# Attention without hi/lo splits: fp32 score matmuls of 64 rows, fp32 value product, three score tiles

## The chip, the cores and the metric

The kernel runs on one core of one Trainium2 chip. The metric is the time of one execution on the device in microseconds (us), lower is better. A core has five engines that run side by side and meet only at semaphores: TensorE (PE in the profile, its weight loads PEld), VectorE (DVE), ScalarE (ACT), GpSimd (POOL) and SyncE (SP), which here only issues the transfers. Matmuls write to PSUM, which has 8 banks; everything else lives in SBUF.

## The reference

```python
# q, k, v: (4 batches, 8 heads, 576 tokens, 64), fp32; tau = 0.02
scores = scale * q @ k.T                              # per batch and head, 576 x 576
thresh = max(scores, axis=-1) - tau
scores = where(scores >= thresh, scores, -1e9)
attn   = exp(scores - max(scores)); attn = attn / (sum(attn) + 1e-9)
x      = attn @ v                                     # -> 2304 tokens x 512
x      = (h - tanh(h)) @ w_out,   h = x @ w_in        # 512 -> 2048 -> 512
out    = (h * sigmoid(h)) @ w_out2, h = x @ w_in2     # 512 -> 2048 -> 512
```

The threshold compares scores with their row's maximum less 0.02, so the scores have to be good to nearly full fp32.

## The kernel before

There are two stages: attention, and then the two feed-forward layers. The feed-forward code (`hidden`, `project`, `chunk`) is the same in both kernels.

**Attention.** The 32 heads are taken in 16 pairs. The two heads of a pair have 2 x 576 query rows, which make nine tiles of 128 rows: eight whole ones (j = 0 to 7, alternately of head 0 and head 1) and a shared one (j = 8) with the last 64 rows of both. Four pairs make a batch of 36 tiles. The code is a software pipeline: each engine has a function `steps`, in which step k does tile k - lag of each kind of work, with lags that are constants (`L_S` = 8 for scores, maximum, statistics and exp; `L_MASK` = 9 for the threshold; `L_NORM` = 11; `L_T` = 13 for transposes; `L_LO` = 14; `L_PV` from 21 for the value product). Each engine runs its own list strictly in this written order, and waits on semaphores where it needs another's result. The first batch is written out, and the other three run in a hardware loop (`Fori`).

**fp32 from fp32r.** PE's one-pass type here is fp32r. An fp32 number is split into a rounded part (hi, by ScalarE's Copy) and the rest (lo, a subtraction by VectorE or GpSimd), and the products of the parts are added in PSUM.

One tile of step k:
- PE, scores (line 833): q_parts holds q hi in rows 0 to 63 and q lo in rows 64 to 127, and k_lo and k_hi are held twice, one copy for each half of the rows. So one tile is four matmuls of 128 rows and 288 columns (two halves `a` of the keys, by k_lo and k_hi); the shared tile has ten. The result is in one of two PSUM tiles `scores` of two banks each, and PE waits for `mask_done` of the tile that had it two tiles ago.
- DVE: maximum over the row (632), threshold and row sum of the tile before (642), statistics for exp (657, two values a row).
- ACT: exp into `probs` (517).
- POOL: `probs` times 1/sum (389), for three tiles at a time, when DVE's reciprocal (698) has come.
- PE, transposes (859): four blocks of 128x128 into one of three PSUM banks `tps`. There are eleven such units in a pair: nine tiles, a "whole" unit for the rest columns of the four even tiles (with j = 7), and a "shared" one of one block. Each bank is emptied by ACT (hi, line 466 and others) and then by DVE (lo, 680; for one unit of eleven by POOL, 397, from a copy `t_raw`), and PE waits for the last of these before it writes the bank again.
- PE, value product (798): per half of the queries 27 matmuls of 288 columns (nine blocks of keys, by lo x hi, hi x lo and hi x hi), spread over four steps as 7, 7, 6, 7; then ACT takes the result (456).

**Loads.** q and k of a pair come into one buffer each (`q_raw`, `k_raw`); SP issues the next pair's (315) when `qk_split` says that all splits of this pair are done. The splits of a pair are made in steps 0 to 5 of its period: ACT's hi (490, 492), POOL's lo (404, 413), and the scores of its first tile wait for them.

The weights of the feed-forward layers are split in the same way by ACT and POOL, in buffers that lie on those of attention; their loads wait for the last split of q and k.

Of the kernel before, what the change touches and what calls it, by code (L numbers as in the profile page):

```python
# [8 lines left out]
F32 = mybir.dt.float32  # L23
F32R = mybir.dt.float32r
ACT = mybir.ActivationFunctionType
AX = mybir.AxisListType
# [15 lines left out]
K_STEPS = (0, 1)  # L42
Q_STEPS = (3, 5)
LATE_STEPS = (2, 3), (4, 5)
THRESHOLD_FIRST = (7,)
FILLING = 18
V_STEPS = (4, 5, 6)
# [12 lines left out]
L_V = L_S + 3  # L60

L_PV = {L_S + 13: (0, 0, 7), L_S + 14: (0, 7, 14), L_S + 15: (0, 14, 20), L_S + 16: (0, 20, 27),
        L_S + 17: (1, 0, 7), L_S + 18: (1, 7, 14), L_S + 19: (1, 14, 20), L_S + 20: (1, 20, 27)}
# [4 lines left out]
LO_BY_POOL = (7,)  # L68
SKIP_AT = 4

# [3 lines left out]
TBANKS = 3  # L74
# [31 lines left out]
def split_in(k, first):  # L106


    p, j = divmod(k, TILES)
    if not 0 <= k < STEPS or (first and p == 0):  # L110
        return None, 0
    keys, queries = LATE_STEPS if first and p == 1 else (K_STEPS, Q_STEPS)
    if j in keys:
        return "keys", keys.index(j)
    if j in queries:
        return "queries", queries.index(j)
    return None, 0


# [17 lines left out]
def by_pool(number):  # L137

    return number % UNITS in LO_BY_POOL


def lows(number):

    pairs, rest = divmod(number + 1, UNITS)
    pool = pairs * len(LO_BY_POOL) + sum(i < rest for i in LO_BY_POOL)
    return pool, number + 1 - pool
# [17 lines left out]

LO_BATCH = PAIRS * len(LO_BY_POOL)

# [7 lines left out]


def pool_view(x, raw, j):

    if j < 2 * FULL:
        return x[:, j % 2, :, j // 2 * P:(j // 2 + 1) * P], raw[:]
    return (x[:].rearrange("p h c s -> p (h c) s")[:, :, FULL * P:SEQ],  # L180
            raw[:].rearrange("p c (h q) -> p h c q", h=2))


def build(nc, q_in, k_in, v_in, tau_in, w_in, out):
    ctx = ExitStack()
    with ctx:
# [23 lines left out]
        att = ExitStack()  # L210

        def asb(name, shape, dt=F32):
            return att.enter_context(nc.sbuf_tensor(name, shape, dt))

        q_raw = asb("q_raw", [P, 2, SEQ])
        k_raw = asb("k_raw", [P, 2, SEQ])
        q_parts = [asb(f"q_parts{u}", [P, 2, 640], F32R) for u in range(2)]
        k_hi = [asb(f"k_hi{u}", [P, 2, SEQ], F32R) for u in range(2)]
        k_lo = [asb(f"k_lo{u}", [P, 2, SEQ], F32R) for u in range(2)]
        v_raw = [asb(f"v_raw{u}", [P, 2, FULL + 1, DH]) for u in range(2)]  # L220
        probs = asb("probs", [P, SLOTS, SEQ])


        v_parts = [asb(f"v_parts{u}", [P, 2, FULL, 3 * DH], F32R) for u in range(2)]
        v_rest = [asb(f"v_rest{u}", [P, 2, 2, DH], F32R) for u in range(2)]
        pT_hi = [asb(f"pT_hi{u}", [P, 2, FULL, SEQ], F32R) for u in range(2)]
        pT_lo = [asb(f"pT_lo{u}", [P, 2, FULL, SEQ], F32R) for u in range(2)]
        t_raw = asb("t_raw", [P, 4, P])
        pR_hi = [asb(f"pR_hi{u}", [P, SEQ], F32R) for u in range(2)]
        pR_lo = [asb(f"pR_lo{u}", [P, SEQ], F32R) for u in range(2)]  # L230
        att.close()


# [6 lines left out]
        g_lo = [sb(f"g_lo{u}", [P, CHUNK], F32R) for u in range(GRING)]  # L240
        w_parts += [sb(f"w_parts{f}", [P, 2, 2, CHUNK], F32R) for f in range(2, FT)]
# [3 lines left out]
        scores = [attp.enter_context(nc.psum_tensor(f"scores{u}", [P, 2, 512], F32)) for u in range(2)]  # L245
# [6 lines left out]
        def v_views(u, i):  # L252

            if i < 2:
                at = slice(2 * i * DH, (2 * i + 1) * DH)
                return v_parts[u][:, 0, :, at], v_parts[u][:, 1, :, at], v_raw[u][:, i, 0:FULL]
            return v_rest[u][:, 0], v_rest[u][:, 1], v_raw[u][:, :, FULL]
# [7 lines left out]
        qk_loaded = sem("qk_loaded")  # L265
        v_loaded = [sem(f"v_loaded{u}") for u in range(2)]
        k_hi_done = sem("k_hi_done")
        q_hi_done = sem("q_hi_done")
        v_hi_done = sem("v_hi_done")
        qk_split = sem("qk_split")  # L270
        v_split = sem("v_split")
# [10 lines left out]
        t_hi_done = sem("t_hi_done")  # L282
        t_copied = sem("t_copied")
        t_lo_by_pool = sem("t_lo_by_pool")
        t_lo_by_dve = sem("t_lo_by_dve")
# [21 lines left out]
        def _(sp):  # L307
            sp.dma_start(tau[:], tau_in).then_inc(tau_loaded, 16)

            def load_qk(B, p):  # L310
                g = PAIRS * B + p
                sp.wait_ge(qk_split, 4 * g)
                for raw, src in ((k_raw, k_in), (q_raw, q_in)):
                    for rows in (slice(0, DH), slice(DH, P)):
                        sp.dma_start(raw[rows], src[:, bass.ds(g * 2, 2), :]).then_inc(qk_loaded, 16)  # L315

            def load_first():

                for h in range(2):
                    for raw, src in ((k_raw, k_in), (q_raw, q_in)):  # L320
                        for rows in (slice(0, DH), slice(DH, P)):
                            sp.dma_start(raw[rows, h], src[:, h, :]).then_inc(qk_first if h == 0 else qk_loaded, 16)

            def load_v(B, p):

                u, g = p % 2, PAIRS * B + p
                if not (isinstance(B, int) and B == 0 and p < 2):
                    sp.wait_ge(v_split, 3 * (g - 1))
                sp.dma_start(v_raw[u][:], v_in[:, bass.ds(g * 2, 2)]).then_inc(v_loaded[u], 16)
# [11 lines left out]
            with sp.Fori(1, BATCH) as B:  # L341
                loads(B, False)
# [6 lines left out]
            sp.wait_ge(qk_split, 4 * PAIRS * BATCH)  # L349
# [19 lines left out]
        def _(pool):  # L369
# [5 lines left out]
            def steps(B, ks, first):  # L375
# [3 lines left out]
                for k in ks:  # L379
# [11 lines left out]
                    for kind, q, number in units_of(k - L_LO, first):  # L391
                        if by_pool(number):
                            u, j, i = q // TILES % 2, q % TILES, lows(number)[0]
                            (hi, raw), (lo, _) = (pool_view(x[u], t_raw, j) for x in (pT_hi, pT_lo))

                            pool.wait_ge(t_copied, LO_BATCH * B + i)
                            pool.tensor_tensor(lo, raw, hi.bitcast(F32),
                                               ALU.subtract).then_inc(t_lo_by_pool, 1)

                    what, h = split_in(k - 1, first)  # L400
                    g, u = PAIRS * B + k // TILES, k // TILES % 2
                    if what == "keys":
                        pool.wait_ge(k_hi_done, 2 * g + h + 1)
                        pool.tensor_tensor(k_lo[u][:, h], k_raw[:, h], k_hi[u][:, h].bitcast(F32),
                                           ALU.subtract).then_inc(qk_split, 1)
                    if what == "queries":
                        pool.wait_ge(q_hi_done, 2 * g + h + 1)

                        if not first or k >= L_NORM:
                            pool.wait_ge(norm_done, STEPS * B + k - L_NORM + 1)  # L410
                        pool.wait_ge(qk_split, 4 * g + 2 + h)
                        rows = q_parts[u][DH:P, h, 0:SEQ]
                        pool.tensor_tensor(rows, q_raw[DH:P, h], rows.bitcast(F32),  # L413
                                           ALU.subtract).then_inc(qk_split, 1)
                        pool.wait_ge(qk_split, 4 * g + 3 + h)
                        pool.sem_inc(pool_waited, 1)

                    q = k - L_V - 1
                    if q % TILES in V_STEPS and here(q):
                        g, u, i = PAIRS * B + q // TILES, q // TILES % 2, q % TILES - V_STEPS[0]  # L420
                        hi, lo, raw = v_views(u, i)
                        pool.wait_ge(v_hi_done, 3 * g + i + 1)
                        pool.tensor_tensor(lo, raw, hi.bitcast(F32), ALU.subtract).then_inc(v_split, 1)

            steps(0, range(STEPS), True)
            with pool.Fori(1, BATCH) as B:
                steps(B, range(STEPS), False)
# [15 lines left out]
        def _(act):  # L443
            def steps(B, ks, first):
# [3 lines left out]
                for k in ks:  # L448
# [9 lines left out]
                    for kind, q, number in units_of(k - L_T, first):  # L458
                        p, j = q // TILES, q % TILES
# [4 lines left out]
                        if kind == "tile":  # L464
                            dst, src = tile_views(pT_hi[u], bank, j)
                            last = act.activation(dst, src, ACT.Copy)
                        elif kind == "whole":
                            last = act.activation(pR_hi[u][:, 0:FULL * P].rearrange("p (t q) -> p t q", t=FULL),
                                                  bank[:], ACT.Copy)
                        else:  # L470
                            for h in range(2):
                                last = act.activation(pR_hi[u][h * DH:(h + 1) * DH, FULL * P:SEQ],
                                                      bank[DH:P, 0, h * REST:(h + 1) * REST], ACT.Copy)
                        last.then_inc(t_hi_done, 1)
# [485 lines left out]
```

## Time and profile before

| | us |
|---|---|
| median of 3 runs | 1238.52 (1236.44 to 1240.39) |
| span of the profiled execution | 1236.2 |
| around the span, by the median | 2.3 |
| attention, to the end of its last value product | 443.4 |
| busy PE, DVE, ACT, POOL | 1134.3, 645.8, 431.8, 315.0 |

The profile gives no other time of the profiled execution than its span, so what lies around it is taken as the median less the span. The page is one execution as the hardware recorded it. Each digit of a row of part 2 is a fortieth of the span, 30.9 us; attention is the first 14. "Idle before" in a row is time in which the engine waited, with the instruction that it waited for. Matmul durations overlap (each has a tail in the array), so the cost of a matmul in a stream is the distance between the starts of two neighbours.

### The profile page before, as it was taken

What the parts mean: (1) busy time and instruction counts of PE and PEld (TensorE: products, weight loads), DVE (VectorE), ACT (ScalarE), POOL (GpSimd) and SP (SyncE); (2) the same over time, 40 slices, a digit from 0 to 9 for tenths busy, and PEclk for the clock granted to TensorE, in tenths of its full rate; (3) what the DMA queues carried; (4) which work ended last, traced back from release to release, by engine and by line L of the source; (5) the groups of instructions that cost most, each with busy time, mean ns of one, the idle gap of its engine ahead of it and who ended that gap; (6) DMA issues with size and microseconds to landing.
All of it is one profiled execution on the core that took longest, in us unless ns stands there. A gap on an engine that the chain in (4) does not pass through costs nothing.

```text
span 1236.2 us, 17043 instructions
## 1 busy us (share of the span) xinstructions
PE 1134.3 (92%) x6032; PEld 967.6 (78%) x6032; DVE 645.8 (52%) x1344; ACT 431.8 (35%) x750; POOL 315.0 (25%) x304
## 2 busy tenths in 40 slices
PE   4787887886888899999999999999999999999998
PEld 3676776775777788888888888997888888888898
DVE  6888987887889956533343433435222232232222
ACT  4666765666767743211111201124221111121111
POOL 2655655665565544200000000006410000000000
PEclk9989998998999999999999999999999999999999
DMA  3232222232222143100000000004300000000000
GB/s 87 56 82 59 50 51 50 59 87 50 49 49 60 34 120 103 52 1 1 1 0 0 0 0 0 1 2 136 99 5 34 1 34 0 0 34 0 0 35 18
DMA packets 15192, 46.31 MB, mean 37 GB/s; under 512 B 2080, under 2 KB 2592, under 8 KB 15136
## 3 DMA queue, kind: packets, MB, share of 16 engines
q1 hardware_dynamic: 15136, 45.62, 13.7%
q8 instruction: 28, 0.46, 0.2%
q14 instruction: 28, 0.23, 0.1%
HBM read 40.89 MB, written 4.72 MB: 37 GB/s over the span
## 4 chain that ended last, share of the span: by engine, by line
PE 67%; DVE 10%; issue 5%; DMA 5%; POOL 2%; SPq 1%; ACT 1%; DVEq 0%; ACTq 0%; POOLq 0%
PE hid L880 32%; PE acc L896 32%; DMA q_raw<-q_in 5%; DVE rowmax L632 3%; DVE probs L642 2%; PE scores L833 2%; DVE stats L657 2%; SPq L315 1%; POOL q_parts L413 1%; PE pv L798 1%; PE tps L859 1%; POOL probs L389 1%; ACT probs L517 1%; DVE pT_lo L680 1%; DVE pR_lo L684 1%
## 5 line engine op out<-in xcount | busy, mean ns | idle before, releaser
L880 PE MATMUL hid<-x_hi,w_parts 128*128 128x512 f32 (+1 forms) x1280 | 384.8, 368 | 2.3 <-DVE x_lo L717 2.1
L896 PE MATMUL acc<-g_hi,w_parts 128*128 128x512 f32 (+1 forms) x1280 | 384.1, 368 | 0.0
L880 PEld LDWEIGHTS hid<-x_hi,w_parts 128*128 128x128 f32 x1280 | 234.0, 188 | 42.9 <-DVE x_lo L717 2.2
L896 PEld LDWEIGHTS acc<-g_hi,w_parts 128*128 128x128 f32 x1280 | 234.3, 189 | 40.0
L880 PE MATMUL hid<-x_lo,w_parts 128*128 128x512 f32 (+1 forms) x640 | 235.4, 368 | 0.0
L896 PE MATMUL acc<-g_lo,w_parts 128*128 128x512 f32 (+1 forms) x640 | 235.4, 368 | 0.0
L731 DVE CAST g_hi<-h_act 128x512 fp32r<-128x512 f32 (+1 forms) x160 | 70.4, 440 | 270.8 <-ACT h_act L560 268.1
L833 PE MATMUL scores<-k_lo,q_parts 128*128 128x288 f32 x336 | 111.2, 352 | 77.6 <-DVE probs L642 65.1
L433 POOL TENSOR_TENSOR w_parts<-w_raw,w_parts 128x1024 fp32r<-128x1024 f32 x30 | 73.4, 2449 | 397.5 <-ACT w_parts L536 397.5
L726 DVE TENSOR_TENSOR h_act<-hid,h_act 128x512 f32<-128x512 f32 (+1 forms) x80 | 51.1, 638 | 205.8 <-ACT h_act L557 205.8
L389 POOL TENSOR_SCALAR probs<-probs,rinv 128x576 f32<-128x576 f32 x144 | 108.6, 758 | 170.7 <-DVE rinv L698 167.4
L833 PEld LDWEIGHTS scores<-k_lo,q_parts 128*128 128x128 f32 x336 | 67.9, 205 | 106.7 <-DVE probs L642 95.7
L557 ACT ACTIVATE h_act<-hid 128x512 f32<-128x512 f32 (+1 forms) x80 | 44.4, 555 | 292.4 <-PE hid L880 292.4
L560 ACT ACTIVATE h_act<-hid 128x512 f32<-128x512 f32 (+1 forms) x80 | 44.4, 555 | 290.6 <-PE hid L880 290.5
L517 ACT ACTIVATE probs<-scores,stats,escale 128x576 f32<-128x576 f32 x144 | 119.7, 831 | 60.5 <-DVE stats L657 60.3
L880 PEld LDWEIGHTS hid<-x_lo,w_parts 128*128 128x128 f32 x640 | 120.8, 189 | 20.0
L896 PEld LDWEIGHTS acc<-g_lo,w_parts 128*128 128x128 f32 x640 | 120.6, 188 | 19.9
L642 DVE SCALAR_TENSOR_TENSOR probs<-scores,stats,probs 128x576 f32<-128x576 f32 x144 | 116.6, 810 | 33.9 <-ACT probs L517 33.3
L859 PE MATMUL tps<-ident,probs 128*128 128x128 f32 x656 | 111.2, 300 | 13.9 <-DVE pT_lo L680 8.2
L733 DVE TENSOR_TENSOR g_lo<-h_act,g_hi 128x512 fp32r<-128x512 f32 (+1 forms) x160 | 120.9, 756 | 5.5
L798 PE MATMUL pv<-pT_hi,v_parts 128*128 128x288 f32 x512 | 122.5, 313 | 0.0
L632 DVE TENSOR_REDUCE rowmax<-scores 128x1 f32<-128x576 f32 x144 | 108.6, 754 | 25.8 <-issue 11.7
(59 smaller groups left out, 1127.6 us busy)
## 6 DMA issues: line engine op xcount, KB each, us to landing
w_raw<-w_in SPq DMA_DIRECT2D x32, 512.0 KB, 3.6
k_raw<-k_in SPq DMA_DIRECT2D x30, 288.0 KB, 4.1
q_raw<-q_in SPq DMA_DIRECT2D x30, 288.0 KB, 5.4
v_raw<-v_in SPq DMA_DIRECT2D x16, 320.0 KB, 5.6
out<-xT SPq DMA_DIRECT2D x4, 1024.0 KB, 4.2
k_raw<-k_in SPq DMA_DIRECT2D x4, 144.0 KB, 2.9
q_raw<-q_in SPq DMA_DIRECT2D x4, 144.0 KB, 3.0
out<-xT SPq DMA_DIRECT2D x1, 512.0 KB, 2.9
```

What stands on the lines that cost most here:

```text
L389: pool.tensor_scalar(tile, tile, r, 1.0, ALU.mult, ALU.mult).then_inc(norm_done, 1)
L433: pool.tensor_tensor(w_parts[f][:, 1], w_raw[f % 2][:], w_parts[f][:, 0].bitcast(F32), ALU.subtract).then_inc(w_split, 1)
L517: act.activation(probs[:, slot_of(q), :].rearrange("p (a s) -> p a s", a=2), scores[q % 2][:, :, 0:HALF], ACT.Exp, bias=stats[:, c, 0:1], ...
L632: dve.tensor_reduce(rowmax[:, c:c + 1], scores[q % 2][:, :, 0:HALF], AX.XY, ALU.max).then_inc(max_done, 1)
L642: dve.scalar_tensor_tensor(out=tile, in0=scores[q % 2][:, :, 0:HALF], scalar=stats[:, c, 1:2], in1=tile, op0=ALU.is_ge, op1=ALU.mult, accu ...
L731: dve.tensor_copy(g_hi[s][:, 0:w], g).then_inc(g_hi_done, 1)
L733: dve.tensor_tensor(g_lo[s][:, 0:w], g, g_hi[s][:, 0:w].bitcast(F32), ALU.subtract).then_inc(g_split, 1)
L798: last = pe.matmul(pv[:, 0:HALF], *todo[i], start=(i == 0), stop=(i == len(todo) - 1))
L833: last = pe.matmul(scores[q % 2][:, a, c0:c0 + w], rows, keys, start=(i == 0), stop=(i == len(todo) - 1))
L859: last = pe.matmul(bank[:, c, :], block, ident[:], is_transpose=True, start=True, stop=True)
L880: last = pe.matmul(hid[f % HBANKS][:, 0:w], a, b[:, kc, 0:w], start=(kc == 0 and i == 0), stop=(kc == KC - 1 and i == 2))
L896: last = pe.matmul(acc[n][:, 0:w], a, b[f % GRING][:, 0:w], start=(f == 0 and i == 0), stop=(f == FT - 1 and i == 2))
```

## The change

q, k, v and the transposed probabilities are no longer split: they are plain fp32, and the matmuls on them are fp32 matmuls. The layer code keeps its splits.

- Scores: q and k are both held twice, in rows 0 to 63 and 64 to 127. The first half of the keys is multiplied from rows 0 to 63, the second from rows 64 to 127, in turn, so a tile is two matmuls of 64 rows and 288 columns. The score tiles are three, not two (six banks).
- The transposes have one bank, not three. Each unit waits until the one before it is copied out. Ten of eleven units are copied by ACT, the "whole" unit (number 8) by DVE, at the place in DVE's step where the lo parts were made, one step after the transposes. Where a step has two units, the value product comes between them.
- Value product: 9 fp32 matmuls per half, as 2, 2, 2, 3.
- q, k and v have two buffers each, loaded when the pair before the last is done with them; no split waits stand before the scores.
- POOL keeps only the scaling of `probs`. The loops over batches are written out.

```diff
-K_STEPS = (0, 1)
-Q_STEPS = (3, 5)
-V_STEPS = (4, 5, 6)
-L_PV = {L_S + 13: (0, 0, 7), L_S + 14: (0, 7, 14), L_S + 15: (0, 14, 20), L_S + 16: (0, 20, 27), ...
+L_PV = {L_S + 13: (0, 0, 2), L_S + 14: (0, 2, 4), L_S + 15: (0, 4, 6), L_S + 16: (0, 6, 9), ...
-LO_BY_POOL = (7,)
+BY_DVE = (8,)
+SBUFS = 3
-TBANKS = 3
+TBANKS = 1
@@ sync
             def load_qk(B, p):
-                g = PAIRS * B + p
-                sp.wait_ge(qk_split, 4 * g)
+                u, g = p % 2, PAIRS * B + p
+                if not (isinstance(B, int) and B == 0 and p < 2):
+                    sp.wait_ge(scores_done, TILES * (g - 1))
-            with sp.Fori(1, BATCH) as B:
+            for B in range(1, BATCH):
-            sp.wait_ge(qk_split, 4 * PAIRS * BATCH)
             load_w(0, 0)
@@ vector
                     for kind, q, number in units_of(k - L_LO, first):
-                        if by_pool(number):
+                        if not by_dve(number):
                             continue
-                        dve.wait_ge(t_hi_done, UNITS * PAIRS * B + number + 1)
+                        dve.wait_ge(t_done, UNITS * PAIRS * B + number + 1)
...
+                            dve.tensor_copy(pR[u][:, 0:FULL * P].rearrange("p (t q) -> p t q", t=FULL),
+                                            bank[:]).then_inc(t_by_dve, 1)
@@ tensor
-                            todo = [(v_parts[u][:, v, c, h * DH:h * DH + P], x[u][:, h, c, cols])
-                                    for c in range(FULL) for h in range(2)
-                                    for v, x in ((0, pT_lo), (1, pT_hi), (0, pT_hi))]
+                            todo = [(v_main(u, c, h), pT[u][:, h, c, cols]) for c in range(FULL) for h in range(2)]
+                            todo += [(v_all[u][:, FULL * 3 * DH:], pR[u][:, cols])]
-                        if not first or q >= 2:
-                            pe.wait_ge(mask_done, n - 1)
+                        if not first or q >= SBUFS:
+                            pe.wait_ge(mask_done, n - SBUFS + 1)
+                                rows = slice(a * DH, (a + 1) * DH)
+                                todo[a] += [(flat[rows, at], k_all[u][rows, h, k0:k0 + w], c0, w) for c0, k0, w in cols]
+                        for i in range(max(map(len, todo))):
+                            for a in range(2):
+                                if i < len(todo[a]):
+                                    rows, keys, c0, w = todo[a][i]
+                                    last = pe.matmul(scores[q % SBUFS][:, a, c0:c0 + w], rows, keys,
+                                                     start=(i == 0), stop=(i == len(todo[a]) - 1))
-                    for kind, q, number in units_of(k - L_T, first):
+                    for i, (kind, q, number) in enumerate(units_of(k - L_T, first)):
+                        if i == 1:
+                            product(k)
                         ...
-                            if by_pool(before):
-                                pe.wait_ge(t_copied, LO_BATCH * B + lows(before)[0])
+                            if by_dve(before):
+                                pe.wait_ge(t_by_dve, DVE_BATCH * B + taken(before)[0])
                             else:
-                                pe.wait_ge(t_lo_by_dve, (UNITS * PAIRS - LO_BATCH) * B + lows(before)[1])
+                                pe.wait_ge(t_by_act, ACT_BATCH * B + taken(before)[1])
-                    product(k)
+                    if len(units_of(k - L_T, first)) < 2:
+                        product(k)
```

## Rows read from the trace of the kernel before

**Rows 1.** The page: span, busy time of the engines, granted TensorE clock by slice.
```profile
span 1236.2 us, 17043 instructions
PE 1134.3 (92%) x6032; PEld 967.6 (78%) x6032; DVE 645.8 (52%) x1344; ACT 431.8 (35%) x750; POOL 315.0 (25%) x304
PEclk9989998998999999999999999999999999999999
```

**Rows 2.** Stretches: each engine's busy us (instructions), granted clock, DMA share, GB/s.
```profile
220.00:240.00 20.00, 16.08 (x101) 13.74 (x101) 17.00 (x42) 13.27 (x24) 11.39 (x13) 0.91 0.31 75
430.00:1236.00 806.00, 798.38 (x3907) 677.41 (x3907) 283.32 (x466) 151.59 (x257) 76.97 (x34) 1.00 0.08 26
```

**Rows 3.** Waits from 30 to 420 us: us in total, times, longest.
```profile
POOL probs L389 <- DVE rinv L698: 140.5, 45, 8.8
PEld scores L833 <- DVE probs L642: 86.3, 114, 6.5
...
ACT probs L517 <- DVE stats L657: 49.8, 74, 3.1
...
ACT k_hi L490 <- DMA q_raw<-q_in: 39.5, 14, 3.7
```

**Rows 4.** Timeline of DVE: start, us, line, operation, idle before.
```profile
198.14 0.76 DVE L632 TENSOR_REDUCE rowmax<-scores 128x1 f32<-128x576 f32 x1 [5.78 <-issue]
...
219.64 0.68 DVE L680 TENSOR_TENSOR pT_lo<-tps,pT_hi 128x512 fp32r<-128x512 f32 x1
220.43 0.76 DVE L632 TENSOR_REDUCE rowmax<-scores 128x1 f32<-128x576 f32 x1
221.10 0.81 DVE L642 SCALAR_TENSOR_TENSOR probs<-scores,stats,probs 128x576 f32<-128x576 f32 x1
221.84 0.22 DVE L657 SCALAR_TENSOR_TENSOR stats<-stat_scale,rowmax,stat_bias 128x2 f32<-128x2 f32 x1
...
246.14 0.76 DVE L632 TENSOR_REDUCE rowmax<-scores 128x1 f32<-128x576 f32 x1
```

**Rows 5.** Timeline of all engines, 279 to 285 us: a threshold, statistics, exp, copy.
```profile
279.29 0.82 DVE L642 SCALAR_TENSOR_TENSOR probs<-scores,stats,probs 128x576 f32<-128x576 f32 x1 [2.12 <-ACT probs L517]
...
280.03 0.22 DVE L657 SCALAR_TENSOR_TENSOR stats<-stat_scale,rowmax,stat_bias 128x2 f32<-128x2 f32 x1
...
280.28 0.83 ACT L517 ACTIVATE probs<-scores,stats,escale 128x576 f32<-128x576 f32 x1
...
284.60 0.60 ACT L466 ACTIVATE pT_hi<-tps 128x512 fp32r<-128x512 f32 x1
```

**Rows 6.** Timeline of PE, its matmuls, three places.
```profile
254.90 0.40 PE L833 MATMUL scores<-k_lo,q_parts 128*128 128x288 f32 x1 [2.67 <-DVE probs L642]
...
283.91 0.66 PE L859 MATMUL tps<-ident,probs 128*128 128x128 f32 x4
284.33 0.39 PE L798 MATMUL pv<-pT_lo,v_parts 128*128 128x288 f32 x1
284.56 0.42 PE L798 MATMUL pv<-pT_hi,v_parts 128*128 128x288 f32 x2
...
285.60 0.40 PE L833 MATMUL scores<-k_lo,q_parts 128*128 128x288 f32 x1
285.83 0.30 PE L833 MATMUL scores<-k_hi,q_parts 128*128 128x288 f32 x1
...
286.23 1.05 PE L859 MATMUL tps<-ident,probs 128*128 128x128 f32 x5
...
439.83 0.29 PE L798 MATMUL pv<-pT_lo,v_parts 128*128 128x288 f32 x1
...
443.44 0.39 PE L880 MATMUL hid<-x_hi,w_parts 128*128 128x512 f32 x1
```

**Rows 7.** Timeline of the start: the first scores and the first maximum.
```profile
8.55 0.58 PE L833 MATMUL scores<-k_lo,q_parts 128*128 128x288 f32 x1 [8.55 <-DVE q_parts L707]
...
10.75 0.76 DVE L632 TENSOR_REDUCE rowmax<-scores 128x1 f32<-128x576 f32 x1
```

More of the change, by code:

```diff
@@ L134, in units_of, with by_dve, taken @@
     return found
-def by_pool(number):
-    return number % UNITS in LO_BY_POOL
-def lows(number):
+def by_dve(number):
+    return number % UNITS in BY_DVE
+def taken(number):
     pairs, rest = divmod(number + 1, UNITS)
-    pool = pairs * len(LO_BY_POOL) + sum(i < rest for i in LO_BY_POOL)
-    return pool, number + 1 - pool
+    dve = pairs * len(BY_DVE) + sum(i < rest for i in BY_DVE)
+    return dve, number + 1 - dve
 def bank_of(number):
@@ L240, in build, with asb @@
         g_lo = [sb(f"g_lo{u}", [P, CHUNK], F32R) for u in range(GRING)]
+        att = ExitStack()
+        def asb(name, shape, dt=F32):
+            return att.enter_context(nc.sbuf_tensor(name, shape, dt))
+        q_all = [asb(f"q_all{u}", [P, 2, 640]) for u in range(2)]
+        k_all = [asb(f"k_all{u}", [P, 2, SEQ]) for u in range(2)]
+        probs = asb("probs", [P, SLOTS, SEQ])
+        v_all = [asb(f"v_all{u}", [P, VCOLS]) for u in range(2)]
+        pT = [asb(f"pT{u}", [P, 2, FULL, SEQ]) for u in range(2)]
+        pR = [asb(f"pR{u}", [P, SEQ]) for u in range(2)]
+        att.close()
         w_parts += [sb(f"w_parts{f}", [P, 2, 2, CHUNK], F32R) for f in range(2, FT)]
         attp = ExitStack()
[L245 removed]
+        scores = [attp.enter_context(nc.psum_tensor(f"scores{u}", [P, 2, 512], F32)) for u in range(SBUFS)]
         tps = [attp.enter_context(nc.psum_tensor(f"tps{u}", [P, 4, P], F32)) for u in range(TBANKS)]
@@ L264, in build @@
         qk_first = sem("qk_first")
-        qk_loaded = sem("qk_loaded")
+        qk_loaded = [sem(f"qk_loaded{u}") for u in range(2)]
         v_loaded = [sem(f"v_loaded{u}") for u in range(2)]
[L267 to L271, printed above, removed]
         scores_done = sem("scores_done")
@@ L389, in steps @@
                         pool.tensor_scalar(tile, tile, r, 1.0, ALU.mult, ALU.mult).then_inc(norm_done, 1)
-                    for kind, q, number in units_of(k - L_LO, first):
-                        if by_pool(number):
[L393 to L423, printed above, removed]
             steps(0, range(STEPS), True)
-            with pool.Fori(1, BATCH) as B:
+            for B in range(1, BATCH):
                 steps(B, range(STEPS), False)
@@ L517, in steps @@
                         act.activation(probs[:, slot_of(q), :].rearrange("p (a s) -> p a s", a=2),
-                                       scores[q % 2][:, :, 0:HALF], ACT.Exp, bias=stats[:, c, 0:1],
+                                       scores[q % SBUFS][:, :, 0:HALF], ACT.Exp, bias=stats[:, c, 0:1],
                                        scale=escale[:]).then_inc(exp_done, 1)
-            for h in range(2):
-                act.wait_ge(qk_loaded if h else qk_first, 64)
-                act.activation(k_hi[0][:, h], k_raw[:, h], ACT.Copy).then_inc(k_hi_done, 1)
-                act.activation(q_parts[0][:, h, 0:SEQ], q_raw[:, h], ACT.Copy).then_inc(q_hi_done, 1)
             steps(0, range(STEPS), True)
-            with act.Fori(1, BATCH) as B:
+            for B in range(1, BATCH):
                 steps(B, range(STEPS), False)
@@ L603, in _ @@
             for u in range(2):
-                dve.memset(q_parts[u][:, 0, SEQ:640].bitcast(F32), 0.0).then_inc(consts_ready, 1)
-                for part in range(2):
-                    dve.memset(v_parts[u][:, part, :, DH:2 * DH].bitcast(F32), 0.0).then_inc(consts_ready, 1)
+                dve.memset(q_all[u][:, 0, SEQ:640], 0.0).then_inc(consts_ready, 1)
             dve.wait_ge(tau_loaded, 16)
@@ L641, in threshold @@
                         tile = probs[:, slot_of(q), :].rearrange("p (a s) -> p a s", a=2)
-                        dve.scalar_tensor_tensor(out=tile, in0=scores[q % 2][:, :, 0:HALF],
+                        dve.scalar_tensor_tensor(out=tile, in0=scores[q % SBUFS][:, :, 0:HALF],
                                                  scalar=stats[:, c, 1:2], in1=tile, op0=ALU.is_ge,
@@ L698, in steps @@
                         dve.reciprocal(rinv[:, cols], rowsum_e[:, cols]).then_inc(rinv_done, 1)
-            for h in range(2):
-                dve.wait_ge(k_hi_done, h + 1)
-                dve.tensor_tensor(k_lo[0][:, h], k_raw[:, h], k_hi[0][:, h].bitcast(F32),
-                                  ALU.subtract).then_inc(qk_split, 1)
-                dve.wait_ge(q_hi_done, h + 1)
-                rows = q_parts[0][DH:P, h, 0:SEQ]
-                dve.tensor_tensor(rows, q_raw[DH:P, h], rows.bitcast(F32), ALU.subtract).then_inc(qk_split, 1)
             steps(0, range(STEPS), True)
-            with dve.Fori(1, BATCH) as B:
+            for B in range(1, BATCH):
                 steps(B, range(STEPS), False)
@@ L860, in steps @@
                         last.then_inc(t_done, 1)
-                    product(k)
+                    if len(units_of(k - L_T, first)) < 2:
+                        product(k)
             steps(0, range(STEPS), True)
-            with pe.Fori(1, BATCH) as B:
+            for B in range(1, BATCH):
                 steps(B, range(STEPS), False)
```

173 lines of the change are left out of this document (47 added, 126 removed).

## The prediction

> **What bounds the kernel now.** I read the page first. PE is busy 92% of the span [rows 1], but that is a mean over two stages. The table of stretches parts them: from 430 us on PE is busy for 798 of 806 us at the full clock, while in attention it has 16.1 of 20 us at a mean granted clock of 0.91, and DVE has 17.0 [rows 2]. The feed-forward stage is bound by PE, its code is the same, and I cost it at no change. So the whole question is attention, which ends at 443.4 us (row 443.44, the first `hid` matmul behind the last value product [rows 6]).
>
> The list of waits says what sets its pace. PE's weight loads for the scores stood 86.3 us for DVE's threshold, exp stood 49.8 us for DVE's statistics, and POOL 140.5 us for DVE's reciprocal [rows 3]: all wait for DVE. The timeline of DVE shows a step: maximum 0.76, threshold 0.74 up to where the statistics start, statistics 0.22, lo part 0.68 [rows 4], 2.4 us. On top of that each pair has a bubble: ACT stood 39.5 us for the transfer of q in 14 pairs [rows 3], since the load goes into a single buffer only after the splits, and PE stood 2.67 us at one such place [rows 6]. Two starts of maximum that are a pair apart give the pair's length: 246.14 - 220.43 = 25.7 us [rows 4], where nine steps of 2.4 would be 21.6. The loop over batches costs 5.78 us at its back edge [rows 4], twice.
>
> **What goes.** DVE loses the lo part in ten of eleven units (0.68 each), ACT the splits of q, k and v, POOL all but its scaling; the load bubble goes, since the buffers are double and the load is released nearly a pair ahead; the back edges go, -11.6 us in all, where I take the written-out code to be fetched in time (if not, some of that comes back). The start gets shorter: the first scores waited at 8.55 us for the split of q [rows 7], and the data were there about 2.4 us earlier, because a copy and the subtractions of the first key and query lie between; -2.4 us.
>
> DVE's own floor is then a chain: threshold 279.29 to 280.03, statistics to 280.25, exp 280.28 to 281.11, and the next threshold [rows 5], some 1.85 us, with the next maximum (0.76) beside exp. With the sums and reciprocals it is about 2.0 us a step, 18 us a pair. The third score tile allows PE to be that far ahead. What is late next is PE.
>
> **What PE pays.** All its prices come from rows 6, at full clock. A value matmul of 288 columns: from 439.83 to 443.44 there are 27, so 0.134 each. The first matmul of a group takes 0.23 (285.60 to 285.83, and 284.33 to 284.56), so 0.10 more. Four transposes take 0.42 (283.91 to 284.33). Before, a pair was 42 x 0.134 for scores, 54 x 0.134 for the product, 41 x 0.105 for transposes and 17 group starts: 5.6 + 7.2 + 4.3 + 1.7 = 18.8 us of 25.7; PE had room.
>
> The price of a plain fp32 matmul is not in this trace. Its ends: below, 288 columns at the transposes' fp32 rate, 0.105/128 x 288 = 0.24 us (even 0.134 if it cost what fp32r does). Above, four passes each with a weight load that nothing covers, 4 x (0.134 + 0.105) = 0.95 us. I take 0.53: the kernel's own code shows that the array takes one split part of each operand in a pass, the full product has four part products, and 4 x 0.134 = 0.53, the loads being covered as they are now. (The Trainium skill, page FP8 and Floating Point Precision, section TensorE Precision Notes, says that true fp32 is four passes through the array; no row here shows it. By that rule the term is 0.53 too.)
>
> Value product: 18 x 0.53 + 8 x 0.10 = 10.4 us a pair, against 8.0 before. Transposes: unchanged, 4.3. Scores: the two matmuls of 64 rows lie in different halves of the array. If they run wholly side by side, a tile costs 0.53 + 0.10, the pair (ten tiles' worth, as the shared tile is double) 6.2; if one behind the other, 11.5. No row shows two matmuls side by side, so I keep both ends and take a third of the second one as uncovered, nearer to the full overlap: 6.2 + 10 x 0.18 = 8.0. (The Trainium skill, page TensorEngine Tiling (Array Packing), section Key Properties, says that a change of tiling mode drains TensorE. That speaks against this change: there are two such changes in every step, and the 0.10 of a group start, which is between groups of one mode, would be too little.)
>
> **The new stall.** With one transpose bank a unit waits for the copy of the one before. Mostly that copy is long done (0.60 by ACT [rows 5], one step ago). Twice a pair it is not. (1) "whole" follows tile 7 in the same step, and that step has no product between them: PE waits 0.60 and two hand-overs, 0.7 us. (2) "whole" is copied by DVE, in DVE's next step, behind maximum, threshold and statistics, and that maximum waits for the scores which PE issues in the very step in which tile 8 wants the bank. So PE issues the scores and then stands for 0.76 + 0.74 + 0.22 + a copy of the same bank by DVE, 0.68 as the lo part [rows 4], 2.4 us and hand-overs, 2.5 us. Behind the waiting transposes stand the value product and the next scores, so DVE waits later too. Together 3.2 us a pair, in 16 pairs.
>
> **The clock.** In attention the granted clock is now at times half, 1.2 in place of 2.4 GHz, a mean of 0.91 in the stretch of rows 2; the wait of 2.67 us [rows 6] is the kind of place behind which it falls. The new stall leaves PE two waits (0.7 and 2.5 us) with one score tile between, so I expect it there in two pairs of three. PE is the bound then: a mean of 0.91 over 20 us is 0.09 x 20 = 1.8 us of full clock lost [rows 2], 2.3 in a pair; I take 1.2 us a pair (ends 0 and 2.4).
>
> **The sum.** A pair by PE: 8.0 + 4.3 + 10.4 + 3.2 + 1.2 = 27.1, less 0.2 because the product's first group start lies in the stall: 26.9 us, against 25.7.
> 15 pairs x 1.2 = +18. The last pair had no load bubble before: +1.2 + 2.9 = +4.1. The first pair has no product yet and stays with DVE: -1. Back edges -11.6. Start -2.4. The tail: nine fp32 matmuls for 27, 4.8 for 3.6 us, +1.2; POOL's splits of v between its scalings go, -1.5. Together +6.8 us.
> Span 1236.2 + 6.8 + 2.3 around it = 1245 us (0.5% over the median 1238.5). Within 0.3%, 3.7 us, I call it the same.
>
> **Rivals.**
> - B, the halves wholly side by side and no lost clock. A pair is 26.9 - 1.8 - 1.2 = 23.9: 16 x 3.0 = 48 us less, 1197 us. For it: PE is dense in seven of nine steps, and denser than now. Against: the two waits with little work between. It ends on the faster side, and decides from a pair under 26.4 us on. (The Trainium skill, page TensorE: Matmul & The Clock Gate, section Part 3: Packing small matmuls, has matmuls in different row groups start about 4 ns apart and run together. That is this case; no row of mine shows it.)
> - C, the halves do not overlap: the pair is 26.9 + 10 x 0.35 = 30.4, 16 x 3.5 = 56 us more, 1301 us. For it: matmuls of one queue start in order, and if an fp32 matmul is several passes in the queue, the second half's first pass stands behind the first half's last. Then the change does not do what its halves are for.
> - D, fp32 costs 0.24 a matmul: PE would fall to 26.9 - 28 x 0.29 = 18.8 with its stalls, and DVE sets the pace with 18 + 2.5 = 20.5 us: -6.4 x 16 = -102, 1143 us. For it only the transposes' rate.
> - E, the passes' loads uncovered, 0.95 a matmul: +28 x 0.42 = 11.8 a pair, +188 us, 1433 us. Against: in rows 6 loads hide behind 0.134 us matmuls.
>
> **Numbers.** Chances: forecast 0.36, B 0.30, C 0.19, D 0.08, E 0.07. The forecast's own range is 1228 to 1268 (ends of clock and a quarter or half uncovered). B spreads from 1185 to 1228 (group starts, a copy more or less hidden), C from 1268 to 1312. 1185 to 1312 leaves out D, E and a little of the edges. Faster by over 0.3%: B, D and a tenth of the forecast, 0.41. Same: 0.09. Slower: 0.50.
>
> **What would show it.** Starts of maximum a pair apart: 26.9 us (23.9 in B, 30.4 in C, 20.5 in D). The list of waits: PE `tps` waiting for DVE `pR`, some 2.5 us, 16 times; exp waiting for statistics still there, but with PE's scores behind it; no wait for the q transfer. PE busy in nearly all of a stretch outside the stall. Distance between two value matmuls of 0.53. Two score matmuls of a tile that start together would show the overlap, 0.5 us apart would show C. The half clock behind the stall of each pair. The gap of 5.78 us gone. I am wrong at the root if PE still waits for thresholds in most steps, or if PE's stall for tile 8 isn't there.

## The result and the profile after

The changed kernel takes 1252.09 us (median of 4 runs, 1248.23 to 1252.48), the kernel before 1237.63 in the same session: a ratio of 1.0108 (95% interval 1.0089 to 1.0127). I had said 1245, and gave "slower" a chance of 0.50. The span has grown by 14.5 us (1236.2 to 1250.7), where the sum had 6.8. The profiled execution took 1252.48 us, 1.8 around its span of 1250.7.

The page of the changed kernel: span, busy time, granted clock by slice, the biggest new groups.
```profile
span 1250.7 us, 14996 instructions
PE 1178.0 (94%) x5744; PEld 916.3 (73%) x5744; DVE 555.2 (44%) x1160; ACT 369.0 (30%) x606; POOL 179.5 (14%) x180
...
PEclk8898888888888899999999999999999999999999
...
L509 DVE TENSOR_REDUCE rowmax<-scores 128x1 f32<-128x576 f32 x144 | 108.9, 756 | 148.1 <-PE scores L692 148.1
...
L692 PE MATMUL scores<-k_all,q_all 64*128 64x288 f32 (+2 forms) x672 | 130.3, 479 | 10.6 <-DMA q_all<-q_in 7.4
```
DVE, ACT and POOL have lost 91, 63 and 136 us of work against [rows 1], and the time has grown. DVE now stands 148.1 us for PE's scores: the bound of attention has gone over to PE. The clock reads 8 in nearly every slice of attention (a mean of 0.8 to 0.9 of full speed), against mostly 9 in [rows 1].

The changed kernel's waits from 30 to 450 us (us in total, times, longest).
```profile
DVE rowmax L509 <- PE scores L692: 143.9, 116, 4.5
...
PE tps L720 <- DVE pR L557: 38.1, 16, 2.5
...
PE tps L720 <- ACT pT L380: 14.8, 21, 1.3
...
PEld scores L692 <- DVE probs L519: 5.6, 15, 0.4
```
These answer to [rows 3]: the 86.3 us that PE's weight loads stood for DVE's threshold have come down to 5.6, and ScalarE's waits for the q transfer are gone. In their place are the two waits that the forecast named: for DVE's copy, 16 times, 2.5 us the longest, and the shorter one for ScalarE's copy.

The changed kernel's PE over some two thirds of a pair (start, us, line, operation, count, idle before), then DVE in the stall.
```profile
281.41 0.66 PE L720 MATMUL tps<-ident,probs 128*128 128x128 f32 x4
282.75 0.66 PE L720 MATMUL tps<-ident,probs 128*128 128x128 f32 x4 [0.69 <-ACT pT L380]
283.34 0.76 PE L692 MATMUL scores<-k_all,q_all 64*128 64x288 f32 x4
286.58 1.09 PE L720 MATMUL tps<-ident,probs 128*128 128x128 f32 x4 [2.49 <-DVE pR L557]
287.46 2.13 PE L654 MATMUL pv<-pT,v_all 128*128 128x288 f32 x4
289.52 1.33 PE L692 MATMUL scores<-k_all,q_all 64*128 64x288 f32 x4
290.78 1.11 PE L720 MATMUL tps<-ident,probs 128*128 128x128 f32 x4
291.69 1.32 PE L654 MATMUL pv<-pT,v_all 128*128 128x288 f32 x4
...
294.23 1.14 PE L654 MATMUL pv<-pT,v_all 128*128 128x288 f32 x4
295.29 0.76 PE L692 MATMUL scores<-k_all,q_all 64*128 64x288 f32 x4
295.98 0.66 PE L720 MATMUL tps<-ident,probs 128*128 128x128 f32 x4
296.47 1.14 PE L654 MATMUL pv<-pT,v_all 128*128 128x288 f32 x4
297.44 0.65 PE L654 MATMUL pv<-pR,v_all 128*128 128x288 f32 x2
298.02 1.30 PE L692 MATMUL scores<-k_all,q_all 64*128 64x288 f32 x10
299.25 0.66 PE L720 MATMUL tps<-ident,probs 128*128 128x128 f32 x4
```
```profile
284.14 0.76 DVE L509 TENSOR_REDUCE rowmax<-scores 128x1 f32<-128x576 f32 x1 [0.70 <-PE scores L692]
284.82 0.81 DVE L519 SCALAR_TENSOR_TENSOR probs<-scores,stats,probs 128x576 f32<-128x576 f32 x1
...
285.55 0.28 DVE L534 SCALAR_TENSOR_TENSOR stats<-stat_scale,rowmax,stat_bias 128x2 f32<-128x2 f32 x1
285.75 0.68 DVE L557 COPY pR<-tps 128x512 f32<-128x512 f32 x1
```
Read the two together. PE issues the scores at 283.34 and then wants the one transpose bank for tile 8. DVE takes maximum, threshold and statistics first and copies last, until 286.43; PE starts at 286.58. The 0.69 us before the whole unit is there too, at 282.75.

Now look at the distances. From scores to transposes it is 0.69 us at 295.29, but 1.26 at 289.52; the value product took 2.06 us at 287.46 and 1.06 at 294.23. The same work at half the speed: behind the stall PE's clock is down. The table of stretches says it directly (busy us and instructions of PE, PEld, DVE, ACT, POOL, then the granted clock).
```profile
286.00:293.00 7.00, 6.42 (x21) 4.20 (x21) 2.06 (x5) 1.92 (x3) 0.00 (x0) 0.57 0.01 2
293.00:307.00 14.00, 14.00 (x81) 9.20 (x80) 10.04 (x26) 8.82 (x15) 4.37 (x6) 1.00 0.37 85
```
In windows of half a us the granted clock is 1.00 up to 285.0, 0.72 in the next one, 0.50 from 285.5 to 292.0, and 1.00 again from 292.5 on: some 6.8 us at the low level. So it falls while PE still stands, some 1.4 us before PE starts again at 286.58. From 285.5 to 292.0 PE is busy for 5.42 of the 6.5 us; at half speed that work takes about 2.7 us longer than at full speed.

Each fp32 matmul has two records on PE (the tile's two matmuls are `x4`). In the tail, behind the last scores, 12 such records run without a break:
```profile
447.43 3.08 PE L654 MATMUL pv<-pT,v_all 128*128 128x288 f32 x12
450.35 0.65 PE L654 MATMUL pv<-pR,v_all 128*128 128x288 f32 x2
```
(450.35 - 447.43)/12 = 0.243 us a record, 0.487 a matmul. And the starts of maximum, a pair apart, in the changed kernel:
```profile
274.31 0.76 DVE L509 TENSOR_REDUCE rowmax<-scores 128x1 f32<-128x576 f32 x1 [0.63 <-PE scores L692]
...
301.61 0.76 DVE L509 TENSOR_REDUCE rowmax<-scores 128x1 f32<-128x576 f32 x1 [0.63 <-PE scores L692]
```
27.30 us, the same within 0.05 in the twelve pairs from the fourth on, against the 25.7 of [rows 4]. (That one was among the longer of the kernel before: its thirteen pairs without a back edge are 25.1 to 26.5 us, 25.5 in the mean.)

### The profile page after: what moved, and what is told of

Its sections match the earlier page's. It is cut to its first block, busy times and chain, and to the rows that moved or that the text cites. A ratio compares the mean times of both kernels' runs of the same rounds, so it can differ in the third digit from the quotient of the medians.

```text
span 1250.7 us, 14996 instructions
## 1 busy us (share of the span) xinstructions
PE 1178.0 (94%) x5744; PEld 916.3 (73%) x5744; DVE 555.2 (44%) x1160; ACT 369.0 (30%) x606; POOL 179.5 (14%) x180
## 4 chain that ended last, share of the span: by engine, by line
PE 92%; DVE 5%; ACT 2%; issue 0%; DMA 0%; SPq 0%; DVEq 0%; ACTq 0%
PE hid L742 31%; PE acc L758 31%; PE pv L654 12%; PE scores L692 9%; PE tps L720 8%; DVE probs L519 2%; DVE rowmax L509 2%; ACT pT L380 1%; ACT probs L402 1%; DVE pR L557 1%; DVE stats L534 0%; DVE x_lo L576 0%; DMA q_all<-q_in 0%; ACT x_hi L425 0%; ACT w_parts L416 0%
## 5 line engine op out<-in xcount | busy, mean ns | idle before, releaser
L720 PE MATMUL tps<-ident,probs 128*128 128x128 f32 x656 | 123.5, 314 | 55.8 <-DVE pR L557 38.1
L509 DVE TENSOR_REDUCE rowmax<-scores 128x1 f32<-128x576 f32 x144 | 108.9, 756 | 148.1 <-PE scores L692 148.1
L720 PEld LDWEIGHTS tps<-ident,probs 128*128 128x128 f32 x656 | 79.0, 156 | 119.3 <-POOL probs L335 51.1
L654 PE MATMUL pv<-pT,v_all 128*128 128x288 f32 x512 | 161.3, 443 | 0.0
L335 POOL TENSOR_SCALAR probs<-probs,rinv 128x576 f32<-128x576 f32 x144 | 105.8, 751 | 335.8 <-DVE rinv L565 335.8
L692 PE MATMUL scores<-k_all,q_all 64*128 64x288 f32 (+2 forms) x672 | 130.3, 479 | 10.6 <-DMA q_all<-q_in 7.4
L592 DVE TENSOR_TENSOR g_lo<-h_act,g_hi 128x512 fp32r<-128x512 f32 (+1 forms) x160 | 127.2, 795 | 5.5
```

Of the source, the lines that this page charges most:

```text
L335: pool.tensor_scalar(tile, tile, r, 1.0, ALU.mult, ALU.mult).then_inc(norm_done, 1)
L509: dve.tensor_reduce(rowmax[:, c:c + 1], scores[q % SBUFS][:, :, 0:HALF], AX.XY, ALU.max).then_inc(max_done, 1)
L592: dve.tensor_tensor(g_lo[s][:, 0:w], g, g_hi[s][:, 0:w].bitcast(F32), ALU.subtract).then_inc(g_split, 1)
L654: last = pe.matmul(pv[:, 0:HALF], *todo[i], start=(i == 0), stop=(i == len(todo) - 1))
L692: last = pe.matmul(scores[q % SBUFS][:, a, c0:c0 + w], rows, keys, start=(i == 0), stop=(i == len(todo[a]) - 1))
L720: last = pe.matmul(bank[:, c, :], block, ident[:], is_transpose=True, start=True, stop=True)
```

## The experiments

The first four ran on one chip, the next three on another and the last on a third, each time with the kernel before beside them. Ratios are to that kernel. The diffs are shortened. A "theory" and a "rival" are what was expected before the run, with the time that each would give.

**1. DVE's copy at the head of its step.**
```diff
                 for k in ks:
+                    for kind, q, number in units_of(k - L_LO, first):   # the copy of the whole unit
+                        ...
                     for part in (maximum, threshold): part(k)
                     ...
-                    for kind, q, number in units_of(k - L_LO, first):
-                        ...
```


> The changed kernel with one thing moved: VectorE's copy of the whole unit stands at the head of its step, ahead of maximum, threshold and statistics. Theory (the stall for tile 8 and the half clock behind it are one thing): PE's wait of 2.49 us before tile 8's transposes goes, and with it the 6.8 us at half clock, 3.4 us of PE's work. A pair falls from 27.3 to about 21.4 us, 16 pairs make -94: 1158 us. Rival (the clock falls in every pair for another reason, such as the 64-row matmuls or the wait of 0.69 us): only the stall goes, a pair is 24.9, and the time 1213 us with the granted clock of attention as low as before.

Measured: 1182.48 us, ratio 0.9564 (0.9548 to 0.958). PE, and the stretch 220 to 360 us:
```profile
263.74 0.66 PE L720 MATMUL tps<-ident,probs 128*128 128x128 f32 x4 [0.69 <-ACT pT L380]
264.32 0.76 PE L692 MATMUL scores<-k_all,q_all 64*128 64x288 f32 x4
265.27 0.63 PE L720 MATMUL tps<-ident,probs 128*128 128x128 f32 x4 [0.19 <-DVE pR L537]
```
```profile
220.00:360.00 140.00, 134.55 (x745) 85.89 (x744) 104.52 (x268) 85.74 (x139) 41.30 (x57) 1.00 0.28 70
```
The stall of 2.49 us is 0.19, the clock is 1.00 over the whole stretch, and a pair is 22.43 us (22.42 to 22.44 from the third on). The theory had 21.4: it took the stall and 3.4 us of clock off 27.3. The stall accounts for 2.30, so the clock was worth 27.30 - 22.43 - 2.30 = 2.57 us, not 3.4. The 3.4 was half of all 6.8 us at the low clock, but some 1.4 of them lie in the stall, where PE has no work to slow down; the 2.7 us worked out above fits. The time missed the theory's 1158 by 24 us: besides the 1.0 us a pair, the theory took the full gain in all 16 pairs, where the first three gain 0 (23.95 for 23.94 us), 3.5 and 3.9 us. The rival (1213, the clock as low as before) is out. One copy moved makes the slower kernel one that is 4.4% faster than the kernel before.

**2. Work for PE in the stall.**
```diff
+                        if kind == "tile" and j == 2 * FULL and here(k - L_S):
+                            ...
+                            for _ in range(5):
+                                pe.matmul(pv[:, 0:HALF], q_all[w][:, 0, 0:P], k_all[w][:, 0, 0:HALF], start=True, stop=True)
                         if kind == "tile":
                             pe.wait_ge(norm_done, STEPS * B + q + 1)
```


> The changed kernel with the stall left as it is, but PE works in it: five fp32 matmuls of 128 rows and 288 columns (5 x 0.485 = 2.4 us) go into the idle value bank before the transposes of tile 8; what they give is never used. Theory: the wait is the same, but the clock stays full: a pair falls by the 3.4 us lost at half clock, 27.3 to 23.9, -54 in all: 1198 us. Rival (the half clock isn't caused by PE's idleness there): no gain, 27.3 or a little more a pair, 1252 to 1256 us.

Measured: 1218.03 us, ratio 0.9846 (0.983 to 0.9863). PE of this kernel, where line 706 is the added work:
```profile
289.31 0.76 PE L693 MATMUL scores<-k_all,q_all 64*128 64x288 f32 x4
289.99 2.69 PE L706 MATMUL pv<-k_all,q_all 128*128 128x288 f32 x10
292.55 0.63 PE L728 MATMUL tps<-ident,probs 128*128 128x128 f32 x4
293.01 1.14 PE L655 MATMUL pv<-pT,v_all 128*128 128x288 f32 x4
```
```profile
220.00:360.00 140.00, 136.56 (x737) 88.66 (x738) 95.21 (x245) 78.17 (x127) 37.18 (x51) 1.00 0.28 68
```
PE reaches tile 8's transposes as late as before (3.24 us behind the scores, against 3.24 in the changed kernel), but the next product takes 1.07 in place of 2.06 us (the scores behind it start at 294.08). With 75 fp32 matmuls more, the kernel is 34 us faster than the changed one. A pair is 24.73 us (24.72 or 24.73 from the third on): 2.57 less than 27.30, the same number as from the first experiment by another way. So the half clock comes from PE's idleness in the stall and not from the 64-row or fp32 matmuls, nor from the wait of 0.69 us alone, which is still there. The size was again expected too large (a pair of 23.9, 1198 us), by the same count of 3.4.

**3. Both halves from the same rows.**
```diff
-                                rows = slice(a * DH, (a + 1) * DH)
+                                rows = slice(0, DH)
```


> The changed kernel with both halves of the keys multiplied from rows 0 to 63 of the array, so that they can't run side by side; the result is the same. Theory (the halves overlap wholly, a fp32 matmul is two of 0.243 us): +0.485 us for each of ten tiles' worth a pair, +4.9 us, +78 in all: 1330 us. Rival (the halves were only partly side by side, or weights were the limit): +1 to +3 us a pair, 1268 to 1300 us. If PE's denser work kept the clock up, up to 27 us less in either.

Measured: 1330.86 us, ratio 1.0761 (1.0727 to 1.0794), 79 us over the changed kernel and as the theory had it (1330). PE:
```profile
267.30 1.23 PE L692 MATMUL scores<-k_all,q_all 64*128 64x288 f32 x4
268.47 0.66 PE L720 MATMUL tps<-ident,probs 128*128 128x128 f32 x4
```
From scores to transposes it is 1.17 us, against 0.69: the 0.48 that one fp32 matmul costs. So in the changed kernel the two halves lie wholly side by side, and my third uncovered was wrong. PE's stall for tile 8 is 2.41 us in every pair here, yet the pairs come as 30.83, 30.78 and 33.97 us in turn: the clock does not cost the same in each.

**4. Three transpose banks, two score tiles.**
```diff
-SBUFS = 3
+SBUFS = 2
-TBANKS = 1
+TBANKS = 3
```


> The changed kernel with PSUM divided as in the kernel before: three banks for transposes, two score tiles. Theory: both bank waits go (0.69 and 2.49 us a pair) and the half clock with them; with two score tiles a step is scores 0.69, maximum 0.76, threshold 0.74 and hand-overs, 2.3 us, as long as PE's own step of 2.25: a pair of 20.7 to 21.5 us, 1145 to 1160 us. Rival (the third score tile is what lets PE be the bound): PE waits for thresholds again in most steps, 2.7 us a step, a pair of 24 to 25 us, 1200 to 1215 us.

Measured: 1183.83 us, ratio 0.9573 (0.9556 to 0.9589), between the two theories. PE:
```profile
264.52 0.76 PE L692 MATMUL scores<-k_all,q_all 64*128 64x288 f32 x4
265.21 1.09 PE L720 MATMUL tps<-ident,probs 128*128 128x128 f32 x8
266.87 0.76 PE L692 MATMUL scores<-k_all,q_all 64*128 64x288 f32 x4 [0.57 <-DVE probs L519]
```
The two units of a step go back to back (`x8`), no bank is waited for. PE waits for the threshold, 0.57 us in the step without a product and some 0.1 in others: steps of 2.35 for 2.25, a pair of 22.64 us. The granted clock from 220 to 360 us is 1.00. So the bank waits are gone by another way, with nearly the time of experiment 1.

**5. The loop written out in the kernel before.**
```diff
-            with dve.Fori(1, BATCH) as B:
+            for B in range(1, BATCH):
```
(on all five engines)

> The kernel before with one part of the change alone: the loop over batches written out. Theory (my term of the sum): the two gaps of 5.78 us at the back edges go and nothing comes in their place, -11.6 us, 1226 us. Rival: code that isn't in the loop has to be fetched, and gaps of the same kind stay: 1234 to 1240 us.

Measured: 1228.03 us, ratio 0.9935 (0.9916 to 0.9954), a gain of 5.7 to 10.4 us. The pairs that had held the gap are 25.25 and 25.48 us long, for 30.46 and 29.91 before: 9.6 us together. So the term was 8 to 10, not 11.6: a part of DVE's two idle times of 5.8 us was, as I read it, load bubble that those pairs have anyway. (The spans of the two profiled executions are 11.7 us apart, 1236.2 and 1224.5, but these are one execution each, and that of the kernel before was 2.7 us over the median here.)

**6. The first experiment, and the last chunk of the product one step on.**
```diff
-        L_S + 17: (1, 0, 2), L_S + 18: (1, 2, 4), L_S + 19: (1, 4, 6), L_S + 20: (1, 6, 9)}
-L_OUT = {L_S + 17: 0, L_S + 21: 1}
+        L_S + 17: (1, 0, 2), L_S + 18: (1, 2, 4), L_S + 19: (1, 4, 6), L_S + 21: (1, 6, 9)}
+L_OUT = {L_S + 17: 0, L_S + 22: 1}
```


> The kernel of the first experiment (VectorE's copy at the head of its step) with the last chunk of the value product, three matmuls, moved one step on, between tile 7's transposes and the whole unit's, where PE now waits 0.69 us for ScalarE's copy. Theory: the wait goes and nothing else changes on PE, a pair of 22.43 falls to 21.75 us, -11 us in all: 1171 us. Rival (the result of that chunk comes a step later, and the next product waits for ScalarE to take it): the gain turns into a wait in front of the next product, 1178 to 1186 us.

Measured: 1173.27 us, ratio 0.9487 (0.9472 to 0.9503), a pair of 21.72 us. PE:
```profile
255.49 0.63 PE L720 MATMUL tps<-ident,probs 128*128 128x128 f32 x4 [0.16 <-ACT pT L380]
255.96 1.14 PE L654 MATMUL pv<-pT,v_all 128*128 128x288 f32 x4
256.93 0.65 PE L654 MATMUL pv<-pR,v_all 128*128 128x288 f32 x2
257.42 0.60 PE L720 MATMUL tps<-ident,probs 128*128 128x128 f32 x4
```
The three matmuls at 255.96 and 256.93 now stand between tile 7's transposes and the whole unit's (257.42), so tile 7's copy runs under them. In place of 0.69 us there is a wait of 0.16 ahead of tile 7, and none in front of the next product. The theory (1171) holds.

**7. Two score tiles alone.**
```diff
-SBUFS = 3
+SBUFS = 2
```


> The changed kernel with two score tiles in place of three, all else the same, one transpose bank too. Theory (the third tile is worth only the hand-over of a threshold to the next scores): 0.1 us in seven steps of a pair, since the kernel with three banks showed 2.35 where the changed one has 2.25 us: +0.5 to +0.7 a pair, 1260 to 1265 us. Rival (with the stall in the pair PE lives on the third tile to catch up): over 1 us a pair, 1270 us or more.

Measured: 1244.76 us, ratio 1.0072 (1.0055 to 1.0089): not slower than the changed kernel's 1.0108 but, if anything, a little faster (the intervals just touch; the medians are 7 us apart), which neither the theory (1260 to 1265) nor the rival (1270 or more) had. Starts of maximum, pairs apart:
```profile
218.68 0.76 DVE L509 TENSOR_REDUCE rowmax<-scores 128x1 f32<-128x576 f32 x1 [0.81 <-PE scores L692]
...
243.90 0.76 DVE L509 TENSOR_REDUCE rowmax<-scores 128x1 f32<-128x576 f32 x1 [0.81 <-PE scores L692]
...
270.74 0.76 DVE L509 TENSOR_REDUCE rowmax<-scores 128x1 f32<-128x576 f32 x1 [0.81 <-PE scores L692]
```
The pairs are of two kinds, 25.22 and 26.84 us. The short one is 0.49 us over the 24.73 of experiment 2, which lost nothing to the clock; the theory had put the second score tile at 0.5 to 0.7. The long one (nine of the twelve from the fourth on are 26.8 to 26.9) has lost 1.6 us to the clock, and the changed kernel's pairs 2.57, every one. From 220 to 360 us the mean clock is 0.96, against 0.88 in the changed kernel:
```profile
220.00:360.00 140.00, 121.92 (x638) 75.98 (x637) 88.78 (x235) 74.19 (x118) 35.92 (x50) 0.96 0.27 67
```
The stall is the same in both:
```profile
256.38 0.71 PE L720 MATMUL tps<-ident,probs 128*128 128x128 f32 x4 [2.49 <-DVE pR L557]
```
Behind it the clock is 0.50 from 257.0 to 260.0 only, and 1.00 from 261.0 on; after the stall before it, which ends at 231.16, it stays at 1.00. In the changed kernel it is low from 285.5 to 292.0. So the same stall costs less here, and in one pair of four nothing; why was not tried. That the length or the phase of PE's period decides it is a guess. The third score tile gives 0.1 us in some steps and is not what the change lives on.

**8. The sixth, and maximum ahead of threshold from the first tile on.**
```diff
-FILLING = 18
+FILLING = 0
```


> The kernel with the product moved, and in the first ten tiles VectorE takes the maximum ahead of the threshold of the tile before, as it does in the later ones. Theory (the first pair runs at VectorE's chain of statistics, exp, threshold, maximum, 2.65 us a tile, and with three score tiles the maximum can lie beside exp): 1.9 to 2.0 us a tile in the first nine, -6 us: 1167 us. Rival (the first scores come too slowly at half clock, or the stages behind them just wait longer): within 2 us of 1173 us.

Measured: 1167.82 us (median of 5), ratio 0.9435 (0.9421 to 0.9449). The first nine tiles take 17.6 us in place of 24.0. This version beats both kernels, by 5.6% and 6.7%.

Not tested: the kernel before with double buffers for q and k alone. What the load bubble is worth by itself, apart from the rest of the change, stays open.

## Why the prediction was right, step by step

The direction and the mechanism held, and the time is inside the own range of the likeliest case (1228 to 1268). The size did not hold as well: +6.8 us of span were forecast, +14.5 measured. Inside the sum for a pair two terms were off, in opposite directions:

| of a pair, us | forecast | measured | from |
|---|---|---|---|
| scores | 8.0 | 6.75 | 8 x 0.69 + 1.23 |
| transposes and product, less 0.2 | 14.5 | 14.8 | the rest of 21.55 |
| PE's work at full clock | 22.5 | 21.55 | 22.43 - 0.69 - 0.19, experiment 1 |
| the two bank waits | 3.2 | 3.18 | 0.69 + 2.49 |
| half clock | 1.2 | 2.57 | experiments 1 and 2 |
| pair | 26.9 | 27.3 | |

- **What bounds it.** Right. DVE, freed of the lo parts, waits for PE.
- **The fp32 matmul, 0.53.** Measured 0.487, or 3.6 times the 0.134 of an fp32r matmul [rows 6]; the estimate was 9% too high. (The Trainium skill, page FP8 and Floating Point Precision, section TensorE Precision Notes, has true fp32 as four passes through the array. The total is near that, and the trace shows a matmul as two records, not as four.)
- **The scores, a third uncovered.** This step was wrong and put the term 1.25 us a pair too high: experiment 3 shows the full overlap. From scores to transposes there are 0.69 us: 0.487, 0.10 for the group start, and 0.10 more, and with both halves in one row group the same 0.20 is left (1.17 less 2 x 0.487). The second 0.10 would fit the drain at a change of tiling mode that the Trainium skill (page TensorEngine Tiling (Array Packing), section Key Properties) has, but no run here parts it from another cause. On the way from 128 rows to 64 there is no such extra: 1.06 us from 294.23 to 295.29, less 4 x 0.243, leaves 0.09, the usual group start. (The overlap is what the Trainium skill, page TensorE: Matmul & The Clock Gate, section Part 3: Packing small matmuls, says; experiment 3 agrees, for fp32 too.)
- **The stall for tile 8.** 2.5 forecast, 2.49 measured, 0.7 and 0.69 for the other. Both came from following the written order of two engines, with no new number.
- **The clock.** The mis-sized term: 1.2 for 2.57 us a pair, 22 us of the time too little if taken in all 16 pairs. The forecast had the fall "in two pairs of three"; in the profiled execution it came in every pair from the fourth on, and the 7 us from 286 on have a mean of 0.57. The price was scaled from the mean of 0.91 in [rows 2], a stretch of the kernel before, in which DVE set the pace; the changed kernel has a mean of 0.88 from 220 to 360 us, and now PE is the bound, so what its work loses goes into the time.
- **The whole span.** Read from the starts of maximum, and behind the last of them from the start of the first `hid` matmul behind the last value product (443.44 and 457.73):

| of the span, us | forecast | measured |
|---|---|---|
| start, to the first maximum | -2.4 | -2.9 (10.75 to 7.87) |
| first pair | +0.2 (1.2 - 1) | -1.3 (25.28 to 23.94) |
| pairs 2 to 15, with the back edges | 14 x 1.2 - 11.6 = +5.2 | +12.1 (366.93 to 379.03) |
| last pair, to its last maximum | +4.1 | +5.4 (19.68 to 25.05) |
| tail | +1.2 - 1.5 = -0.3 | +1.0 (20.80 to 21.84) |
| feed-forward stage | 0 | +0.2 |
| sum | +6.8 | +14.5 |

  The middle row holds most of the miss. Its pairs are 27.07 us in the mean for 25.5 before, so each grew by 1.55 and not 1.2, because the 25.7 of [rows 4] was too long a base and the pair too short a forecast; and the back edges gave 8 to 10 for 11.6. The tail had no bank waits in the forecast; the trace has them there too, 0.69 and 0.88 us.
- **The rivals.** B was right in its first half (the halves side by side) and wrong in its second (no lost clock). Taken alone, the error of the scores would have put the forecast 20 us too high (16 x 1.25), and that of the clock 22 us too low (16 x 1.37). The forecast of 1245 is nearer to 1252 than its terms deserve, and that is luck. C is experiment 3, priced at 1301 and measured at 1331: a pair was priced at 30.4 and is 31.9 in the mean, since there too the clock cost more than I gave it. D and E are out by 0.487 us for a matmul, where they need 0.24 and 0.95.

## What to carry to other kernels

When a change takes work off three engines and puts it on the fourth, look at the waits that the fourth gets, not at the work taken away: here 70 us (1252 to 1182) lay behind one copy that was last in its engine's step. With a single buffer between two engines, write down for each user what stands ahead of the release in the other engine's list, and whether that in turn waits for the first engine. And where PE is the bound, count a stall of a few us as the stall and up to once more for the clock behind it (2.30 and 2.57 us here, but 0 or 1.6 for the same stall in experiment 7); if the stall can't go, work that nobody needs can be cheaper than idling.

## What the runs showed of the hardware that I had not expected

- Five useless fp32 matmuls (ten records, 2.4 us) in the stall of each pair made the kernel 34 us faster, 1252.1 to 1218.0: the stall stayed, and the granted clock from 220 to 360 us rose from 0.88 to 1.00.
- The clock fell inside the stall, some 1.4 us before PE had work again, so 6.8 us at the low clock cost 2.57 us and not 3.4.
- The same stall does not always cost the same: 2.49 us cost 2.57 us more in each pair of 27.3, but in the kernel with two score tiles, whose pairs differ by 0.5 us of work, 1.6 us in three pairs of four and nothing in the others; and in experiment 3 the pairs with one stall of 2.41 us are 30.8, 30.8 and 34.0 us. What decides it was not tried.
- Two fp32 matmuls of 64 rows in the two halves of the array run side by side at no loss, each in two records: 0.69 against 1.17 us from scores to transposes.
